# The x loads of the last four batches move from SP's DMA queue to ACT's

## The chip, the cores and the metric

One core of one Trainium2 chip runs the kernel. The metric is the device time of one execution in microseconds, lower is better.

## The reference

Three layers follow one another; everything is float32.

```python
def _attn_ref(x, state):              # x (8, 8, 512, 64), state (8, 8, 32, 64)
    scores = scale * x @ state^T      # softmax over the 32 state rows
    xread = a @ state
    scores2 = scale * state @ x^T     # softmax over the 512 rows of x
    sread = a2 @ x                    # the slot reads
    return concatenate([xread, sread], axis=2)

def _moe_ref(x, phi, w1, w2):         # x (4608, 512), 32 slots, 8 experts
    logits = x @ phi
    d = softmax of logits over the tokens;  slot_input = d.T @ x
    slot_out[e] = relu(slot_input[e] @ w1[e]) @ w2[e]
    c = softmax of logits over the slots;   return c @ slot_out

def _moe2_ref(x, w_gate, w_output_gate, w1, w2):   # top 1 of 8 experts, two gates
    out[mask] = gate_w * eom * (relu(x[mask] @ w1[e]) @ w2[e])
```

## The kernel before, in words

**Stages.** Attention comes first, one batch of x (1 MB) per step. Then the sums over tokens of the first expert layer, its eight matrices w1 and its eight w2 (2 MB each), then the gates and the sorting of tokens by expert of the second layer, and last a loop over 34 to 41 tiles of 128 tokens, with the second layer's matrices held in SBUF. The kernel is written with one hand-ordered program per engine (SP, GpSimd, TensorE, ScalarE = ACT, VectorE) and semaphores between them. There is no planner: each engine's order is the order of its code.

**Buffers.** `arena` and `parts` hold ten slots of 2 MB. x uses the slots 6 and 7 as four buffers `x_sb[0..3]` (a batch b is in buffer b % 4), so x of batch 4 may be loaded when batch 0 has been read for the last time. The last reader is TensorE's `slot_reads` (line 604), which counts up `rd_psum`; the other reader is the copy of x into the layout `xr` (line 288, `lay_x`, on VectorE for batches 0 and 1, on GpSimd from 2 on), which counts up `x_laid`. The matrices of the first expert layer are numbered u = 0 to 15 (w0 to w15 here), those of the second from 16 on. w0 to w3 have slots that nothing used before, w4 waits for `rd_psum` of 6, w5 for the last scores, w6 for `rd_psum` of 8, w7 for the last logits, w8 and w9 for `u_psum`, which TensorE gives behind attention; from w10 on each waits until its slot's matrix has been used. The first eight are loaded in four pieces of 512 KB, in which each of 128 partitions gets 4 KB at a stretch. A load of x has stretches of 1 KB, the state loads (`load_state`, line 293, eight of 64 KB) of 256 B.

**One step k of attention.** TensorE turns the scores of batch k - 2 (`turn_scores`, lines 565 and 571, two halves), turns x of batch k (`turn_x`, line 541, four groups of four transposes), turns the weights of batch k - 3 (line 582), computes the scores of batch k - 1 (line 554), the logits of batch k - 3 (line 589) and the slot reads of batch k - 2 (line 604). ACT in step k: for each of two halves the copy of the turned scores of batch k - 2 out of PSUM (line 905) and two copies of turned x (line 911); then exponentials (921), the logits' copy (927), and the exponential and the copy of the scores of batch k - 1 (938, 942). TensorE needs `xr` of batch k for line 541, GpSimd makes it with line 288 as soon as x has landed and the four groups of the batch before have been turned. GpSimd's line 432 (the normalised weights of batch k - 2) stands behind line 288 of batch k + 1.

**SP** issues nearly all loads, in one order:

```python
            load_w(0)
            load_x(4)
            load_w(1)
            load_x(5)
            load_w(2)
            for i in range(2):
                load_state(e, i)
            load_x(6)
            load_w(3)
            load_x(7)
            e.wait_ge(rd_psum, NB - 2)
```

`load_x(b)` waits, for b of 4 to 7, for `rd_psum` and `x_laid` of b - 3, and so everything behind it on SP waits too. ACT issues one DMA in the whole kernel before the change, the table of tokens (line 1006).

Of the kernel before, what the change touches and what calls it, by code (L numbers as in the profile page):

```python
# [27 lines left out]
NB, NH, S, NS, D = 8, 8, 512, 32, 64  # L28
# [3 lines left out]
J = S // P  # L32
# [22 lines left out]
def last_user(u):  # L55

    before = [v for v in range(u) if SLOT[v] == SLOT[u]]
    return before[-1] if before else None


def build(nc, x, state, phi, w1, w2, wgate, wogate, v1, v2, out, table):
    with ExitStack() as ctx:
# [3 lines left out]
        def sem(name):  # L66
            return ctx.enter_context(nc.semaphore(name))
# [8 lines left out]
        def slot(k):  # L76
            if k < NE:
                return arena[:, k * UNIT:(k + 1) * UNIT]
            return parts[:, (NE + 1 - k) * UNIT:(NE + 2 - k) * UNIT]


        x_sb = [arena[:, 6 * UNIT + 2048 * q:6 * UNIT + 2048 * (q + 1)] for q in range(4)]
# [103 lines left out]
        x_laid, gates_in = sem("x_laid"), sem("gates_in")  # L186
        small_in, phi_in, rows_in = sem("small_in"), sem("phi_in"), sem("rows_in")
        x0_in, x0_laid, x_in = sem("x0_in"), sem("x0_laid"), [sem(f"x_in{q}") for q in range(4)]
# [10 lines left out]
        rd_psum, lgt_psum, lgt_copied = sem("rd_psum"), sem("lgt_psum"), sem("lgt_copied")  # L199
# [41 lines left out]
        def pieces(u):  # L241

            return 4 if u < EARLY else 1
# [46 lines left out]
        def load_state(e, i):  # L290

            for g in range(G):
                e.dma_start(state_n[32 * g:32 * g + 32, :, 64 * i:64 * i + 64],
                            state[:, 2 * g + i, :, :].rearrange("b n d -> n b d")).then_inc(small_in, 16)
# [9 lines left out]
        def wait_used(e, u):  # L304

            if u < 2 * NE:
                e.wait_ge(w_used, u + 1)
            else:
                e.wait_ge(g_psum, u + 1 - 2 * NE)
# [4 lines left out]
        @block.sync  # L314
        def _(e):
            e.dma_start(state_rows, state.rearrange("b h (f t) d -> (b h f) (t d)", f=2)).then_inc(rows_in, 16)
            half = NH // 2
            x0 = x[0].rearrange("h (p j) d -> p h (j d)", j=J)
            x0_sb = x_sb[0].rearrange("p (h c) -> p h c", h=NH)
            e.dma_start(x0_sb[:, 0:half, :], x0[:, 0:half, :]).then_inc(x0_in, 16)  # L320
            e.dma_start(x0_sb[:, half:NH, :], x0[:, half:NH, :]).then_inc(x_in[0], 16)
            e.dma_start(phi_sb[:, :, :], phi.rearrange("(g p) e -> p g e", p=P)).then_inc(phi_in, 16)

            def load_x(b):
                if b >= 4:
                    e.wait_ge(rd_psum, b - 3)
                    e.wait_ge(x_laid, b - 3)
                e.dma_start(x_sb[b % 4].rearrange("p (h c) -> p h c", h=NH),
                            x[b].rearrange("h (p j) d -> p h (j d)", j=J)).then_inc(x_in[b % 4], 16)

            def load_w(u):
                v = last_user(u)
                if v is not None:
                    wait_used(e, v)
                src, ex, _ = w_dram[u]
                rows = src[ex].rearrange("(p c) n -> p (c n)", p=P)
                step = UNIT // pieces(u)
                for a in range(0, UNIT, step):
                    e.dma_start(slot(SLOT[u])[:, a:a + step], rows[:, a:a + step]).then_inc(w_in[SLOT[u]], 16)

            for b in range(1, 4):
                load_x(b)
            e.wait_ge(no_row_ready, 2)
            e.dma_start(table[0:FIRST_ROW, :], no_row[:, :]).then_inc(table_out, 16)
            e.dma_start(wg_sb[:, :, 0:NE], wgate.rearrange("(p c) e -> p c e", p=P)).then_inc(gates_in, 16)
            e.dma_start(wg_sb[:, :, NE:2 * NE], wogate.rearrange("(p c) e -> p c e", p=P)).then_inc(gates_in, 16)
            load_w(0)
            load_x(4)
            load_w(1)
            load_x(5)  # L350
            load_w(2)
            for i in range(2):
                load_state(e, i)
            load_x(6)
            load_w(3)
            load_x(7)
            e.wait_ge(rd_psum, NB - 2)
            e.wait_ge(x_laid, NB - 2)
            load_w(4)
            e.wait_ge(st_psum, 2 * NB)  # L360
            load_w(5)
            e.wait_ge(rd_psum, NB)
            e.wait_ge(x_laid, NB)
            load_w(6)
            e.wait_ge(lgt_psum, NB)
            load_w(7)
            e.wait_ge(u_psum, 2)
            for u in range(8, NU):
                load_w(u)
            for ex in range(NE):  # L370
                wait_used(e, max(v for v in range(NU) if SLOT[v] == ex))

                if ex >= 2:
                    e.wait_ge(v2_in[ex - 1], 16)
                    e.sem_inc(v2_ready, 1)
                e.dma_start(slot(ex).rearrange("p (c n) -> p c n", c=CF),
                            v2[ex].rearrange("(c p) n -> p c n", p=P)).then_inc(v2_in[ex], 16)
                if ex == 1:
                    e.wait_ge(v2_in[0], 16)
                    e.sem_inc(v2_ready, 1)  # L380
            e.wait_ge(v2_in[NE - 1], 16)
            e.sem_inc(v2_ready, 1)
# [508 lines left out]
        def _(e):  # L891
# [5 lines left out]
            for k in range(STEPS):  # L897
                for i in range(2):
                    if 0 <= k - 2 < NB:

                        m = 2 * (k - 2) + i
                        e.wait_ge(e2_psum, m + 1)
                        if k - 2 >= 1:
                            e.wait_ge(rd_psum, k - 2)
                        e.activation(e2[i], pE[:, :].rearrange("p (j c) -> p j c", j=J), ACT.Copy)\
                         .then_inc(e2_copied, 1)
                    for g in (2 * i, 2 * i + 1) if k < NB else ():
                        e.wait_ge(xt_psum, G * k + g + 1)
                        if k >= 2:
                            e.wait_ge(st_psum, 2 * (k - 1))  # L910
                        e.activation(xT[k % 2][:, g, :], pX[g % 2][:, :], ACT.Copy).then_inc(xt_copied, 1)  # L911
                if k == 2:
                    e.wait_ge(pre_psum, 3)
                    for i in range(2):
                        e.activation(pcat[:, :, i, :], pPhi[i][:, 0:NB * NS].rearrange("p (b e) -> p b e", b=NB),
                                     ACT.Copy, scale=1.0 / SCALE).then_inc(pre_copied, 1)
                for i in range(2):
                    if 0 <= k - 2 < NB:
                        m = 2 * (k - 2) + i
                        e.wait_ge(sub_done, m + 1)  # L920
                        e.activation(ew[i], ew[i], ACT.Exp).then_inc(ew_ready, 1)

                def keep_across(b):
                    e.wait_ge(lgt_psum, b + 1)
                    if b >= 1:
                        e.wait_ge(lg_psum, b)
                    e.activation(lgT, pT[:, 0:P], ACT.Copy).then_inc(lgt_copied, 1)

                if 3 <= k < STEPS - 1:
                    keep_across(k - 3)  # L930
                for i in range(2):
                    if 0 <= k - 1 < NB:
                        b = k - 1
                        m = 2 * b + i
                        e.wait_ge(nb_ready, m + 1)
                        if b >= 1:
                            e.wait_ge(e2_psum, m - 1)
                        e.activation(e2T[i], pS[i][:, :], ACT.Exp, bias=nbias[:, i:i + 1],
                                     accum_out=sum2[:, b, i:i + 1]).then_inc(e2t_ready, 1)
                        if b >= 1:  # L940
                            e.wait_ge(r_psum, m - 1)
                        e.activation(sT[i], pS[i][:, :], ACT.Copy).then_inc(st_copied, 1)
                if k in (NB, STEPS - 1):

                    q = int(k > NB)
                    e.wait_ge(srt_psum, q + 1)
                    e.activation(srT[:, q, :, :].rearrange("p g (b n) -> p b g n", b=4),
                                 pX[q][:, :].rearrange("p (b g n) -> p b g n", b=4, g=G),
                                 ACT.Copy).then_inc(srt_copied, 1)
                if k == STEPS - 1:  # L950
                    keep_across(k - 3)
# [410 lines left out]
```

## Time and profile before

| | |
|---|---|
| time, median of 3 runs | 486.56 us (485.65 to 487.3) |
| profiled execution: its time | 489.24 us |
| profiled execution: span | 487.5 us |
| mean granted TensorE clock | 0.961 |
| TensorE matmul busy | 432.2 us (89%) |
| VectorE, ACT, GpSimd busy | 143.4, 124.1, 123.6 us |
| moved by DMA | 87.27 MB, 179 GB/s over the span |

The profile is one execution. Busy time is that of the matmuls as modelled, and does not show what is waited for; the chain that ended last and the idle time in front of an instruction do. In rows of the timeline the first number is the start in microseconds from the span's start, the second the time from the first of the merged instructions to the end of the last, `x4` their number, and the bracket behind them the idle time of that engine before them with what ended it. SPq is SP's sequencer, which issues DMAs; the time beside it is that of issuing and not of the transfer.

### The profile page before, as it was taken

To read this page: it belongs to the slowest core of one execution; us is meant where nothing else is said; L and a number is where in the kernel's file an instruction comes from. 1 tells how busy PE (TensorE), PEld (TensorE's weight loads), DVE (VectorE), ACT (ScalarE), POOL (GpSimd) and SP (SyncE) were. 2 spreads that over 40 slices of the span, in tenths; PEclk is the share of its full clock that TensorE was granted. 3 is DMA by queue.
4 is the path that set the end of the run, shared out by engine and by line. 5 is a ranking of instruction groups with operands and counts; after the bars stand their busy time and mean duration, and the time that the engine had idled before them with its cause. 6 is when DMAs were issued, how large, how long until landed. Compare 5 with 4: busy or idle time off the path is not lost.

```text
span 487.5 us, 9528 instructions
## 1 busy us (share of the span) xinstructions
PE 432.2 (89%) x3474; PEld 229.3 (47%) x3475; DVE 143.4 (29%) x410; ACT 124.1 (25%) x329; POOL 123.6 (25%) x190
## 2 busy tenths in 40 slices
PE   7869786599877957799999999999999999999991
PEld 5657564474315524444444444444444444444440
DVE  2579789850000782102111110101011110101000
ACT  3868675221000200112112121212112121212100
POOL 2343332104000003023242323323242323323110
PEclk9999999989998858799999999999999999999997
DMA  8979909669999999766782101011010101011110
GB/s 286 285 260 300 346 18 327 219 223 428 429 428 428 428 425 386 272 225 212 244 285 89 45 23 46 23 46 42 26 44 24 46 23 45 23 46 44 23 48 2
DMA packets 31710, 87.27 MB, mean 179 GB/s; under 512 B 6140, under 2 KB 14908, under 8 KB 29628
## 3 DMA queue, kind: packets, MB, share of 16 engines
q1 hardware_dynamic: 27580, 76.66, 42.7%
q0 software_dynamic: 3952, 9.54, 5.9%
q8 instruction: 24, 0.39, 0.3%
q10 hardware_dynamic: 144, 0.59, 0.3%
q14 instruction: 10, 0.08, 0.0%
HBM read 77.27 MB, written 9.78 MB: 179 GB/s over the span
## 4 chain that ended last, share of the span: by engine, by line
PE 70%; DMA 18%; DVE 5%; issue 3%; ACT 1%; POOL 1%; SPq 0%; POOLq 0%; DVEq 0%; ACTq 0%
PE bank L868 51%; DMA arena<-in_moe_w 12%; DMA arena<-in_x 6%; PE bank L855 5%; PE bank L753 3%; PE bank L771 1%; PE bank L541 1%; PE bank L530 1%; PE bank L554 1%; PE bank L848 1%; POOL z L288 1%; PE bank L582 1%; PE bank L804 1%; PE bank L690 1%; PE bank L571 1%
## 5 line engine op out<-in xcount | busy, mean ns | idle before, releaser
L868 PE MATMUL bank<-arena,z 128*128 x560 | 251.9, 603 | 0.0
L868 PEld LDWEIGHTS bank<-arena,z 128*128 128x128 f32 x560 | 104.5, 191 | 123.5 <-issue 119.5
L1321 DVE TENSOR_SCALAR z<-bank 128x256 f32<-128x256 f32 x70 | 26.5, 420 | 222.9 <-PE bank L855 222.9
L1032 ACT ACTIVATE z<-bank,gate_to 128x512 f32<-128x512 f32 x35 | 24.0, 687 | 224.3 <-PE bank L868 224.3
L480 POOL DMA_INDIRECT out<-z,rows_to x35 | 36.1, 1033 | 29.9 <-POOL rows_to L477 29.9
L477 POOL CAST rows_to<-gate_to 128x1 int32<-128x1 f32 x35 | 6.4, 184 | 146.5 <-ACT z L1032 146.5
L460 POOL DMA_INDIRECT z<-token_rows,rows_from x32 | 33.6, 1049 | 25.6 <-POOL rows_from L467 25.6
L804 PE MATMUL bank<-arena,soT 128*32 128x256 f32 x224 | 19.6, 510 | 9.3 <-DMA arena<-in_moe_w 8.5
L855 PEld LDWEIGHTS bank<-cT,parts 32*128 32x128 f32 x560 | 19.2, 189 | 16.7 <-issue 16.6
L855 PE MATMUL bank<-cT,parts 32*128 32x128 f32 x560 | 25.9, 300 | 0.0
L541 PE MATMUL bank<-ident,z 128*128 128x128 f32 x128 | 17.0, 275 | 7.6 <-POOL z L288 5.5
L1024 ACT ACTIVATE z<-bank 128x256 f32<-128x256 f32 x70 | 23.0, 388 | 1.1 <-PE bank L855 1.1
L460 POOL DMA_INDIRECT z<-token_rows,sidx x4 | 4.2, 1054 | 71.5 <-DVE sidx L1290 70.6
L288 POOL COPY z<-arena 128x2048 f32<-128x2048 f32 x6 | 11.4, 1894 | 39.1 <-DMA arena<-in_x 24.9
L432 POOL TENSOR_TENSOR parts<-z,rrec 128x512 f32<-128x512 f32 x16 | 16.4, 1047 | 17.5 <-DVE rrec L1103 17.4
L911 ACT ACTIVATE arena<-bank 128x512 f32<-128x512 f32 x32 | 17.5, 602 | 11.5 <-PE bank L541 11.4
L541 PEld LDWEIGHTS bank<-ident,z 128*128 128x128 f32 x128 | 14.1, 140 | 9.8 <-POOL z L288 6.2
L771 PE MATMUL bank<-arena,z 128*32 128x512 f32 x96 | 12.2, 650 | 5.7 <-DMA arena<-in_moe_w 5.7
L804 PEld LDWEIGHTS bank<-arena,soT 128*32 128x32 f32 x224 | 8.3, 138 | 18.1 <-DMA arena<-in_moe_w 10.5
L530 PE MATMUL bank<-ident 128*128 128x128 f32 x86 | 15.1, 337 | 1.6 <-POOL ident L389 1.6
L530 PEld LDWEIGHTS bank<-ident 128*128 128x128 f32 x86 | 12.9, 179 | 4.0 <-issue 2.5
L753 PE MATMUL bank<-arena,z 128*32 128x512 f32 x128 | 14.1, 594 | 0.0
(202 smaller groups left out, 398.5 us busy)
## 6 DMA issues: line engine op xcount, KB each, us to landing
arena<-in_moe_w SPq DMA_DIRECT2D x21, 2048.0 KB, 21.6
arena<-in_moe_w SPq DMA_DIRECT2D x32, 512.0 KB, 6.9
arena<-in_x SPq DMA_DIRECT2D x7, 1024.0 KB, 6.9
parts<-in_moe_w SPq DMA_DIRECT2D x3, 2048.0 KB, 12.9
arena<-in_x SPq DMA_DIRECT2D x2, 512.0 KB, 5.8
token_rows<-z ACTq DMA_DIRECT2D x1, 578.0 KB
out<-z,rows_to POOLq DMA_INDIRECT x35, 2.9
z<-in_state SPq DMA_DIRECT2D x1, 512.0 KB, 3.5
```

The lines of the kernel that those rows point to most:

```text
L460: e.indirect_dma_start(row[q], None, table, bass.IndirectOffsetOnAxis(ap=rows, axis=0), bounds_check=last_row, oob_is_err=False).then_inc( ...
L480: e.indirect_dma_start(out, bass.IndirectOffsetOnAxis(ap=rows_to[:, q % 2:q % 2 + 1], axis=0), ysb[q % 2], None, bounds_check=last_out, oo ...
L530: e.transpose(to[:, 0:P], ident[:, :], ident[:, :])
L541: mm = e.transpose(pX[g % 2][:, P * j:P * j + P], xr[:, j, P * g:P * g + P], ident[:, :])
L753: mm = e.matmul(pX[fh][32 * c:32 * c + 32, :], siTm[:, P * u + NS * c:P * u + NS * c + NS], w[:, c, 512 * fh:512 * fh + 512], start=(u == ...
L804: mm = e.matmul(pG[ex % 4][32 * q:32 * q + 32, 0:GW], soT[:, c, 0:NS], w[:, c, GW * q:GW * q + GW], start=(c == 0), stop=(c == CD - 1))
L855: mm = e.matmul(bank[g][:, P * h:P * h + P], gNow[p][32 * g:32 * g + 32, P * h:P * h + P], cT[p][32 * g:32 * g + 32, :], start=True, stop= ...
L868: mm = e.matmul(pY[p][:, :], hT[p][:, c, :], arena[:, bass.ds(ex * UNIT + 512 * c, 512)], start=(c == 0), stop=(c == CF - 1))
L911: e.activation(xT[k % 2][:, g, :], pX[g % 2][:, :], ACT.Copy).then_inc(xt_copied, 1)
L1024: a = e.activation(hT[p][:, 2 * g:2 * g + 2, :], bank[g][:, 0:GW].rearrange("p (c t) -> p c t", c=2), ACT.Relu)
L1032: e.activation(ysb[p], pY[p][:, :], ACT.Copy, scale=gate_to[:, q, 0:1])\
L1321: v = e.tensor_scalar(hT[p][:, 2 * g:2 * g + 2, :], bank[g][:, 0:GW].rearrange("p (c t) -> p c t", c=2), 0.0, None, ALU.max)
```

## The change

SP's `load_x` loses its two waits and is called for batches 1 to 3 only. The loads of x of batches 4 to 7 are issued by ACT, in step k = 3 to 6 for batch k + 1, behind the wait for the slot reads of batch k - 3 that ACT has there in any case and before the first copy of line 905; a wait for `x_laid` is added in front of each. SP's order becomes w0, w1, w2, the state loads, w3, then w4 with its waits as before.

```diff
             def load_x(b):
-                if b >= 4:
-                    e.wait_ge(rd_psum, b - 3)
-                    e.wait_ge(x_laid, b - 3)
                 e.dma_start(x_sb[b % 4].rearrange("p (h c) -> p h c", h=NH),
                             x[b].rearrange("h (p j) d -> p h (j d)", j=J)).then_inc(x_in[b % 4], 16)
...
             load_w(0)
-            load_x(4)
             load_w(1)
-            load_x(5)
             load_w(2)
             for i in range(2):
                 load_state(e, i)
-            load_x(6)
             load_w(3)
-            load_x(7)
             e.wait_ge(rd_psum, NB - 2)
...
                         e.wait_ge(e2_psum, m + 1)
                         if k - 2 >= 1:
                             e.wait_ge(rd_psum, k - 2)
+                        if i == 0 and 4 <= k + 1 < NB:
+                            e.wait_ge(x_laid, k - 2)
+                            e.dma_start(x_sb[(k + 1) % 4].rearrange("p (h c) -> p h c", h=NH),
+                                        x[k + 1].rearrange("h (p j) d -> p h (j d)", j=J)).then_inc(x_in[(k + 1) % 4], 16)
                         e.activation(e2[i], pE[:, :].rearrange("p (j c) -> p j c", j=J), ACT.Copy)\
                          .then_inc(e2_copied, 1)
```

## Rows read from the trace of the kernel before

**Rows 1.** The page, part 4: the chain that ended last, by engine.

```profile
PE 70%; DMA 18%; DVE 5%; issue 3%; ACT 1%; POOL 1%; SPq 0%; POOLq 0%; DVEq 0%; ACTq 0%
```

**Rows 2.** That chain in order of time: start us, us, what.

```profile
35.53 6.87 DMA arena<-in_x
...
51.04 11.97 DMA arena<-in_x
...
137.55 36.26 DMA arena<-in_moe_w
```

**Rows 3.** Timeline of TensorE, 34 to 72 us: transposes of x (L541).

```profile
34.83 0.65 PE L604 MATMUL bank<-arena 128*32 128x64 f32 x31 [3.43 <-issue]
...
36.44 1.04 PE L541 MATMUL bank<-ident,z 128*128 128x128 f32 x8
...
44.39 1.09 PE L541 MATMUL bank<-ident,z 128*128 128x128 f32 x8 [0.44 <-POOL z L288]
...
55.27 1.09 PE L541 MATMUL bank<-ident,z 128*128 128x128 f32 x8 [2.98 <-POOL z L288]
...
65.03 1.10 PE L541 MATMUL bank<-ident,z 128*128 128x128 f32 x8 [2.11 <-POOL z L288]
```

**Rows 4.** Timeline of SP, 0 to 200 us: the DMA issues.

```profile
13.78 3.01 SPq L339 DMA_DIRECT2D arena<-in_moe_w  x4
24.38 0.38 SPq L328 DMA_DIRECT2D arena<-in_x  x1
...
35.53 0.38 SPq L328 DMA_DIRECT2D arena<-in_x  x1
...
38.80 8.00 SPq L293 DMA_DIRECT2D z<-in_state  x8
46.90 1.35 SPq L328 DMA_DIRECT2D arena<-in_x  x1
48.29 2.56 SPq L339 DMA_DIRECT2D arena<-in_moe_w  x4
51.04 0.38 SPq L328 DMA_DIRECT2D arena<-in_x  x1
```

**Rows 5.** Timeline of GpSimd, 10 to 100 us: a copy of x (L288).

```profile
53.33 1.89 POOL L288 COPY z<-arena 128x2048 f32<-128x2048 f32 x1 [6.97 <-DMA arena<-in_x]
```

**Rows 6.** Timeline of ACT, 10 to 66 us: line 905, first half, steps 3 to 6.

```profile
25.40 0.65 ACT L905 ACTIVATE arena<-bank 128x512 f32<-128x512 f32 x1
...
36.21 0.60 ACT L905 ACTIVATE arena<-bank 128x512 f32<-128x512 f32 x1 [2.64 <-PE bank L565]
...
44.26 0.63 ACT L905 ACTIVATE arena<-bank 128x512 f32<-128x512 f32 x1
...
52.61 0.62 ACT L905 ACTIVATE arena<-bank 128x512 f32<-128x512 f32 x1
```

**Rows 7.** DMA packets, MB, share: 38 to 40, 46 to 48, 170.5 to 176 us.

```profile
q1 hardware_dynamic: 710, 0.74, 105.8%
...
q1 hardware_dynamic: 1267, 0.39, 126.1%
...
q1 hardware_dynamic: 121, 1.72, 74.2%
q10 hardware_dynamic: 116, 0.54, 23.7%
```

**Rows 8.** Line 328, the x loads of SP: issue (ns min/median/max) and landing.

```profile
L328 SPq DMA_DIRECT2D arena<-in_x x7: 378/602/3375, 2.8 to 51.0; - x7
...
DMA to landing us min/median/max: 6.3/6.9/11.1
```

**Rows 9.** Stretches: length, busy PE PEld DVE ACT POOL, PEclk, DMA share, GB/s.

```profile
20.00:22.00 2.00, 2.00 (x25) 0.92 (x23) 1.38 (x2) 1.69 (x5) 0.89 (x1) 1.00 1.03 416
23.50:25.50 2.00, 1.67 (x30) 1.58 (x30) 1.90 (x6) 2.00 (x7) 1.19 (x2) 1.00 0.05 18
32.00:36.00 4.00, 1.18 (x36) 1.08 (x37) 1.74 (x7) 1.57 (x4) 2.64 (x3) 1.00 0.67 263
...
171.00:173.00 2.00, 0.00 (x0) 0.00 (x0) 2.00 (x12) 0.06 (x1) 0.00 (x0) 1.00 0.99 412
173.00:183.00 10.00, 7.19 (x64) 2.77 (x64) 8.51 (x47) 0.38 (x1) 0.00 (x0) 0.50 1.01 429
```

## The prediction

> **What bounds the kernel now.** I read the page first. The chain that ended last is mostly TensorE (the output matmuls at its end) with 18% DMA in it [rows 1]. Those 18% are of two kinds, which the chain in order of time separates: short pieces in the attention phase, where a transfer of x is waited for, and long ones behind 137 us, where the expert weights are [rows 2]. The change touches the first kind. The weights from the ninth on are requested only when matmuls behind the attention phase have run, so they start later or earlier exactly as that phase ends, and a microsecond won or lost in attention arrives whole at the end.
>
> So the question is when attention ends. Its steps are best read at one instruction, the first transposes of x of a batch (line 541), which stand at 36.44, 44.39, 55.27 and 65.03 us for batches 4 to 7. Ahead of the last three TensorE idled 0.44, 2.98 and 2.11 us for GpSimd's copy of x (line 288) [rows 3]. Without these waits the steps are 7.51, 7.90 and 7.65 us: I take 7.7. The copies themselves waited for the DMA (the queue's own rows are the next to read): TensorE goes on 1.94 us after a copy starts, as 53.33 to 55.27 shows [rows 3, 5].
>
> Why were they late? x6 was issued at 46.90, because SP spent 8.00 us before it on eight small loads of state; ACT reaches its line 905 of that step at 44.26 [rows 4, 6]. x7 was issued at 51.04 behind w3 in the same queue and was not there until 63 [rows 2, 4]. x4 and x5 stand ahead of w1 and w2 in the queue and were nearly in time. A transfer of x that meets nothing takes 6.3 us from issue to landing [rows 8].
>
> **What the change removes.** SP's four waits and four issues go, at 0.38 us or more each [rows 8]; nothing waits for SP itself. The best case follows from the waits alone: 0.44 + 2.98 + 2.11 = 5.5 us, less what the issue on ACT costs.
>
> **What it adds on ACT.** Four issues ahead of the copy of line 905, one in each of the steps that began it at 25.40, 36.21, 44.26 and 52.61 [rows 6]. No row shows a load issued on ACT; the same load took SP 378 ns at least, 602 in the median and 3375 at most, where earlier transfers still filled its queue [rows 8]. A gain of time is excluded, so the cost is 0.38 to 3.4 us each; ACT's queue is empty each time, so I take 0.38. Behind the issue stand the copy and, through it, TensorE's next transposes. For x4 and x5 TensorE will be waiting anyway (below), so these hide; for x6 and x7 I charge 0.1 each. The new waits are old ones or long met (the copy of batch k-3 out of the buffer), and cost nothing.
>
> **What it moves.** x4 goes from 24.38 to 25.4, x5 from 35.53 to 36.2, x6 from 46.90 to some 44, x7 from 51.04 to 52.6 on the old clock. But SP's other loads are moved too, past four waits each: w1, w2, the eight state loads and w3 no longer queue behind an x. SP finished w0's issue at 16.8 [rows 4], so all of them are requested from then on. Before, the DMA engines idled after w0 (18 GB/s from 23.50 to 25.50 [rows 9]) and x4 came first out of the pause. Now w1 stands there, and x4 must share.
>
> How two queues share, the trace shows in one place: 121 packets of SP's queue went beside 116 of ACT's in 5.5 us, 1.72 and 0.54 MB [rows 7]. They alternate packet by packet, whatever the size. That is bad for x: its packets are 1 KB, those of w 4 KB. Per engine (16 of them) a w packet takes 4096 B / (416 GB/s / 16) = 0.158 us [rows 9], an x packet 2 us x 16 / 710 = 0.045 [rows 7], a state packet of 256 B 2 x 16 / 1267 = 0.025 [rows 7]. x has 64 packets per engine, w 32 per matrix of 2 MB, the state loads 128 in all. A turn beside w costs 0.203 us, beside state 0.070.
>
> **x4.** Of the 6.3 us alone, 64 x 0.045 = 2.9 are data; I put 1.9 ahead of them (the pause ended at about that distance from the issue) and 1.5 behind. First packet 25.4 + 1.9 = 27.3. w0 ends about 6.2 us behind its last issue, at 23.0 (the DMA is idle soon after [rows 9]); w1 and w2 of 2.10 MB / 416 GB/s = 5.05 us each would end at 33.1. So 5.8 us or 36 w packets are left: 36 x 0.203 = 7.3, to 34.6. The other 28 go beside state, 2.0, to 36.6. Landing 38.1, TensorE 40.0 in place of 36.44.
>
> **x5.** Issued at 36.2, whatever x4 does (its wait is for the scores and reads of batch 1); first packet 38.1. State packets left then: 128 - 28 - 1.5/0.025 = 40, so 40 x 0.070 = 2.8, to 40.9; 24 go beside w3, 4.9, to 45.8. Landing 47.3, TensorE 49.2; the step alone would allow 40.0 + 7.7 = 47.7.
>
> **x6, x7.** ACT stands at line 905 some 8.0 us behind the first transposes (44.26 - 36.44 = 7.8, 52.61 - 44.39 = 8.2 [rows 3, 6]): x6 at 48.0, when w3 is through. Alone it needs 6.3 + 1.94: 56.2; the step allows 49.2 + 7.7 = 56.9. x7 at 57.2, TensorE 65.4. With 0.1 twice: 65.6 against 65.03.
>
> **Sum:** batch 4 +3.6, batch 5 +4.8, batch 6 +1.6, batch 7 +0.5 us; the two ends of the chain nearly cancel. The profiled execution took 489.24 (span 487.5), so it would read about 489.7; it lies 2.7 above the median of 486.56, and on that median the sum is 487.0. Bounds: x5 needs only 0.8 us less to cost nothing over its step, and an x4 held up by 2 us less brings 2 us; so this case alone covers 485.0 to 489.0.
>
> **Rivals.** (1) *x is hardly held up.* If the weights' packets come slower than I take it once SP's queue is full, or the shared row [rows 7] is no measure for loads, x4 and x5 land as alone: TensorE 36.4 for batch 4, 44.4, 52.7, 60.6 for batch 7, with the issue costs 60.8: 4.2 us faster, 482.3. For it: the waits of rows 3 do go. The Trainium skill (DMA: Bandwidth & Descriptors, Issuing engines are not separate DMA queues) says that starting transfers from several engines saves only the time to issue them, as all interleave on the same engines. By that rule the gain is bounded by x6's 46.90 - 44.26 = 2.6 us, and it speaks against this change; the packet counts above agree with it.
>
> (2) *x5 is the last out of the backlog.* Place: step of batch 5. All data ahead (x5 itself, 100 state packets, w3) ends at 36.6 + 2.9 + 2.5 + 5.05 = 47.1; if x5's packets start by 38.9 or later, state is gone, every turn is beside w3, and it ends there: landing 48.6, TensorE 50.5, batch 7 at 66.9: 1.9 slower, 488.5; with x4 also 1.5 later (a longer start behind a full queue) 490. It decides from where batch 5 starts behind 50.2. The gap of 3.43 us in line 604, which nothing in the profile explains [rows 3] and which fell in w1's transfer, could come a second time and leads to the same side.
>
> (3) *The clock.* TensorE was busy 1.18 of 4 us around that gap and the granted clock stayed 1.00 (2.4 GHz), yet 173 to 183, behind at least 2 us without any matmul, ran at 0.50 (1.2 GHz) [rows 9]. If the longer wait for x4 drops it, the step behind it, 7.5 of 8 us TensorE, stretches by about half of the time at the low level: up to 1.7 us, 488.7. The Trainium skill (TensorE: Matmul & The Clock Gate, Why this matters for your kernels) warns that a gap between bursts throttles the clock again; the first row disagrees, the second agrees.
>
> **Chances.** Forecast 0.50, (1) 0.20, (2) 0.24, (3) 0.06. A measurement of this kernel tells 0.3% (1.5 us) from no change. The forecast's own spread puts 0.2 of it on faster, 0.6 on same, 0.2 on slower: 0.10, 0.30, 0.10. (1) goes to faster but for 0.01. (2) goes to slower but for 0.04, (3) half and half. Faster 0.30, same 0.37, slower 0.33. The range for 8 in 10 runs from (1), 482.3, to (2) with its late x4, 490. The likeliest case's own is 485.0 to 489.0.
>
> **What would show it.** Four loads of x on ACT's queue; SP done with w3's issue before 36. No pause of the DMA behind w0. The copies of line 288 for batches 4 to 7 at about 38, 47, 55 and 63. Batch 4's transposes near 40, the waits for batches 6 and 7 under 1 us. If x4 lands before 35 the sharing is wrong; if batch 4 starts in time and the gain is missing, look at ACT's issues. Behind 65 us every stage must keep its length, or the step that carries attention's time to the end is wrong.

## The result: 1.4% slower

| | before | changed |
|---|---|---|
| time, median | 486.93 us (4 runs) | 493.03 us (4 runs) |
| ratio | | 1.0136, 95% interval 1.0104 to 1.0169 |
| profiled execution: time, span | 489.24, 487.5 us | 492.43, 490.6 us |
| mean granted TensorE clock | 0.961 | 0.958 |

487.0 was predicted, with a range from 482.3 to 490. The kernel lost 6.1 us, and the two profiles differ by 3.2 only. The first experiment clears that up: the profiled execution of before was an unlucky one, with a pause that others don't have.

The profile after, in the order of the prediction's steps. The timeline of SP, 13 to 100 us:

```profile
14.60 8.64 SPq L336 DMA_DIRECT2D arena<-in_moe_w  x12
23.28 14.47 SPq L293 DMA_DIRECT2D z<-in_state  x8
37.80 61.48 SPq L336 DMA_DIRECT2D arena<-in_moe_w  x20
```

w0, w1 and w2 are requested by 23.2 us, the state loads by 37.8 (they took 14.5 us to issue and not 8.0 [rows 4]; in experiment 8, where hardly anything stood in front of them, 4.7). The issues of x on ACT:

```profile
24.98 0.45 ACTq L900 DMA_DIRECT2D arena<-in_x  x1
34.05 0.38 ACTq L900 DMA_DIRECT2D arena<-in_x  x1
51.32 0.37 ACTq L900 DMA_DIRECT2D arena<-in_x  x1
59.85 0.38 ACTq L900 DMA_DIRECT2D arena<-in_x  x1
```

An issue on ACT costs what it does on SP with an empty queue. GpSimd's copies of x for batches 4 to 7:

```profile
40.35 1.89 POOL L288 COPY z<-arena 128x2048 f32<-128x2048 f32 x1 [13.68 <-DMA arena<-in_x]
...
47.67 1.89 POOL L288 COPY z<-arena 128x2048 f32<-128x2048 f32 x1 [3.41 <-PE bank L534]
...
56.70 1.89 POOL L288 COPY z<-arena 128x2048 f32<-128x2048 f32 x1 [3.35 <-DMA arena<-in_x]
...
65.13 1.89 POOL L288 COPY z<-arena 128x2048 f32<-128x2048 f32 x1 [3.25 <-DMA arena<-in_x]
```

x4 took 15.4 us from issue to copy (15.3 to its landing), where 6.3 had been the least from issue to landing [rows 8]; x6 and x7, which meet nothing, took 5.4 and 5.3 to their copies. TensorE's first transposes of x, which answer to [rows 3]:

```profile
42.30 1.97 PE L534 MATMUL bank<-ident,z 128*128 128x128 f32 x8 [7.85 <-POOL z L288]
...
51.61 1.04 PE L534 MATMUL bank<-ident,z 128*128 128x128 f32 x8
...
60.14 1.04 PE L534 MATMUL bank<-ident,z 128*128 128x128 f32 x8
...
68.67 1.04 PE L534 MATMUL bank<-ident,z 128*128 128x128 f32 x8
```

Two things are to be seen. Batch 4 waits 7.85 us and its transposes then take 1.97 us in place of 1.04, at half clock. And from batch 5 on nothing waits for x any more, yet the steps are 8.53 us, twice to the hundredth, not the 7.7 that I had used. What sets them stands in the chain that ended last, between 49 and 55 us (start, us, what):

```profile
49.64 0.68 DVE nbias L1088
50.32 0.62 DVE rsum L1098
...
51.13 0.66 DVE rsum L1098
...
51.98 0.40 DVE rs L1128
...
52.81 0.28 DVE z L1138
53.09 0.61 DVE rmx L1067
...
53.72 0.70 DVE z L1071
...
54.56 0.63 PE bank L564 x4
55.19 0.87 PE bank L534 x8
```

It is VectorE's chain, into which TensorE's four pieces (L564, L534, L575, L547) are strung.

### The profile page after: what moved, and what is told of

It is laid out like the page before. It is cut to its first block, busy times and chain, and to the rows that moved or that the text cites. A ratio compares the mean times of both kernels' runs of the same rounds, so it can differ in the third digit from the quotient of the medians.

```text
span 490.6 us, 9524 instructions
## 1 busy us (share of the span) xinstructions
PE 432.3 (88%) x3474; PEld 229.1 (47%) x3475; DVE 144.1 (29%) x410; ACT 123.8 (25%) x329; POOL 123.6 (25%) x190
## 4 chain that ended last, share of the span: by engine, by line
PE 69%; DMA 17%; DVE 6%; issue 2%; ACT 2%; POOL 1%; SPq 0%; DVEq 0%; POOLq 0%; ACTq 0%
PE bank L861 51%; DMA arena<-in_moe_w 12%; DMA arena<-in_x 5%; PE bank L848 5%; PE bank L746 3%; PE bank L764 2%; PE bank L534 1%; DVE rsum L1098 1%; DVE rmx L1067 1%; PE bank L564 1%; PE bank L547 1%; PE bank L841 1%; PE bank L575 1%; PE bank L683 1%; DVE z L1071 1%
## 5 line engine op out<-in xcount | busy, mean ns | idle before, releaser
L534 PE MATMUL bank<-ident,z 128*128 128x128 f32 x128 | 17.7, 284 | 10.3 <-POOL z L288 7.8
L288 POOL COPY z<-arena 128x2048 f32<-128x2048 f32 x6 | 11.3, 1891 | 38.2 <-DMA arena<-in_x 31.0
L534 PEld LDWEIGHTS bank<-ident,z 128*128 128x128 f32 x128 | 14.9, 146 | 12.0 <-POOL z L288 8.1
L575 PE MATMUL bank<-ident,parts 128*128 128x128 f32 x64 | 10.3, 286 | 5.7 <-DVE z L1138 5.3
L523 PE MATMUL bank<-ident 128*128 128x128 f32 x86 | 13.4, 308 | 1.6 <-POOL ident L382 1.6
```

The costliest lines, as they stand in the source:

```text
L534: mm = e.transpose(pX[g % 2][:, P * j:P * j + P], xr[:, j, P * g:P * g + P], ident[:, :])
```

## The experiments

Two theories stood at the start. **Theory 1:** x4 shares the DMA engines with w1, w2 and the state loads, packet by packet. **Theory 2:** the issue on ACT is what costs. Two side questions: the clock, and the baseline.

**1. The kernel before once more** (no edit, one run).

> The kernel before, unchanged, for a second profile. In the first profile TensorE had an unexplained gap of 3.43 us in line 604 of the fourth step, and that execution took 489.24 us against a median of 486.93. Theory A: the gap is an accident of one execution; here it is under 1.5 us and batch 4's transposes start 2 to 3 us earlier than 36.44, time about 487. Theory B: the gap belongs to the kernel and is here again at 3.4 us.

486.38 us. Theory A holds: line 604 has no such gap, and in none of the twelve other profiles of this study is the gap in front of batch 4 above 1.8 us. TensorE's transposes, batches 4 to 7:

```profile
33.27 1.04 PE L541 MATMUL bank<-ident,z 128*128 128x128 f32 x8
...
41.92 1.09 PE L541 MATMUL bank<-ident,z 128*128 128x128 f32 x8
...
53.50 1.97 PE L541 MATMUL bank<-ident,z 128*128 128x128 f32 x8 [2.67 <-POOL z L288]
...
63.35 1.09 PE L541 MATMUL bank<-ident,z 128*128 128x128 f32 x8 [0.94 <-POOL z L288]
```

An ordinary execution starts batch 4 at 33.3 and batch 7 at 63.4. The changed kernel is late against that by 9.0 us at batch 4 and 5.3 at batch 7, and its time by 492.43 - 486.38 = 6.05. The row of batch 6 shows half clock (1.97 us) behind a wait of 2.67 us; in the first profile the clock had stayed up through the pause of 3.43 and a wait of 2.98 us [rows 3, 9]. So the length of a wait alone doesn't tell whether the clock falls.

**2. x alone.** ACT still issues x4 to x7; SP holds back the rest.

```diff
             load_w(0)
+            e.wait_ge(x_in[3], 32)
             load_w(1)
```

> The changed kernel, but SP waits until x7 has landed before it requests w1, w2, the state loads and w3. ACT still issues x4 to x7. Theory 1 (the loss comes from sharing the DMA engines with w1, w2 and state): x4 lands 6.3 us behind its issue, at about 31.3, batch 4 starts near 33.5, the steps are the 8.53 us that the changed kernel shows when it waits for nothing, batch 7 near 59.5: 9 us earlier than in the changed kernel, about 484 us. Theory 2 (issuing on ACT is what costs): x lands early but the time stays within 2 us of the changed kernel's 493.

482.62 us, ratio to before 0.9904 (0.9869 to 0.9939). x4's copy and the first transposes of batches 4 and 7:

```profile
31.41 1.89 POOL L288 COPY z<-arena 128x2048 f32<-128x2048 f32 x1 [5.21 <-DMA arena<-in_x]
...
34.82 1.04 PE L535 MATMUL bank<-ident,z 128*128 128x128 f32 x8
...
59.23 1.04 PE L535 MATMUL bank<-ident,z 128*128 128x128 f32 x8
```

Theory 2 is out: with the same four issues on ACT the kernel is 10 us faster than the changed one, and faster than before.

**3. SP's old pace.** The two waits in front of each x load come back on SP, without the loads.

```diff
             load_w(0)
+            old_wait(4)    # rd_psum and x_laid of 1, and so on
             load_w(1)
+            old_wait(5)
             load_w(2)
...
+            old_wait(6)
             load_w(3)
+            old_wait(7)
```

> The changed kernel with SP's old waits kept in their old places, without the x loads: w1, w2, w3 are requested when they were before. ACT issues x4 to x7. Theory 1 (sharing): x4 meets w1 alone, all its turns beside 4 KB packets for about 6 us, and lands near 35.5; batch 4 starts near 37.5, x6 meets state and w3. In all 1 to 3 us slower than before, 488 to 490, well ahead of 493. Theory 2 (ACT's issue costs): 492 or more.

496.42 us, 1.0162 (1.0116 to 1.0209), beside 1.0136 (1.0104 to 1.0169) for the changed kernel: not told apart from it by these intervals. Theory 1's number, 488 to 490, missed; taken alone, the time fits theory 2's ("492 or more"). The profile shows that it is not the issue that costs. TensorE's two long waits:

```profile
41.64 1.97 PE L542 MATMUL bank<-ident,z 128*128 128x128 f32 x8 [9.09 <-POOL z L288]
...
65.75 1.97 PE L542 MATMUL bank<-ident,z 128*128 128x128 f32 x8 [6.09 <-POOL z L288]
```

x4, issued at 24.09, was copied at 39.70 and not at 35.5. Its packets had gone sooner; ACT's queue from 24.5 to 34 and from 34 to 36 us:

```profile
q10 hardware_dynamic: 958, 0.97, 34.6%
...
q10 hardware_dynamic: 68, 0.07, 9.3%
```

Those are 1,026 packets. x4 has 1,040, 1,024 of data and one short one on each of the 16 DMA engines, which counts the semaphore up; x5, issued at 32.10, stands behind it in the same queue, so the count alone doesn't say whose they are. The trace's events of x4's semaphore do: 15 of the DMA engines had reported by 35.50 us and the last one at 39.64. One was late by 4 us, and a load has landed when its slowest engine is through. w2 had been requested in SP's queue from 31.3 us on. And x6, issued at 50.67, met w3, which SP had issued at 49.87 on the same event, and was copied at 63.81: 13.1 us where the changed kernel, in which w3 was long through, took 5.4. One matrix in flight in the other queue is enough. ACT's issues took 0.37 to 0.45 us here too, as in experiment 2, so theory 2 gains nothing from the 496.

**4. All on SP, x first.** The same as 2, with who issues x undone.

```diff
             load_w(0)
             load_x(4)
-            load_w(1)
             load_x(5)
-            load_w(2)
-            for i in range(2):
-                load_state(e, i)
             load_x(6)
-            load_w(3)
             load_x(7)
+            load_w(1)
+            load_w(2)
+            for i in range(2):
+                load_state(e, i)
+            load_w(3)
```

> The kernel before, all on SP, with w1, w2, the state loads and w3 moved behind x7; ACT issues nothing. It differs from the run in which x was alone on ACT's queue only in who issues x. If who issues matters little (theory 1), the time is within 2 us of that run's 482.6; x4 is issued when the reads of batch 0 are done, x6 some 2 us earlier than ACT could. If issuing on ACT is itself worth something, this one is slower than that run by 2 us or more.

482.48 us, 0.9905 (0.9883 to 0.9928), equal to experiment 2. Its transposes:

```profile
32.65 1.04 PE L541 MATMUL bank<-ident,z 128*128 128x128 f32 x8
...
41.18 1.04 PE L541 MATMUL bank<-ident,z 128*128 128x128 f32 x8
...
49.71 1.04 PE L541 MATMUL bank<-ident,z 128*128 128x128 f32 x8
...
58.24 1.04 PE L541 MATMUL bank<-ident,z 128*128 128x128 f32 x8
```

No wait for x, and three steps of 8.53 us. The late weights do not show in the time.

**5. w3 ahead of the state loads** (in the changed kernel: `load_w(3)` moved up behind `load_w(2)`; one run).

> The changed kernel with w3 ahead of the state loads. Theory 1a (packets of the two queues alternate one for one, so the size of what x meets decides): all 64 turns of x4 are beside 4 KB packets, 64 x 0.203 = 13.0 us from 28.7, landing near 43 and batch 4 near 45, 2.5 us behind the changed kernel's 42.30. Theory 1b (x4 must let through whatever was requested ahead of it, in bytes): w1 and w2 are ahead in both, so x4 lands at 40.3 as there.

```profile
45.46 1.97 PE L534 MATMUL bank<-ident,z 128*128 128x128 f32 x8 [11.03 <-POOL z L288]
```

x4's copy starts at 43.51 and batch 4 at 45.46; the time is 498.70. Theory 1a had 43 and 45, theory 1b 40.3. What came behind w2 in the other queue decided, though w1 and w2 were ahead in both.

**6. Smaller packets** (in the changed kernel, w1 and w2 in eight pieces; one run, 493.89 us).

```diff
-            return 4 if u < EARLY else 1
+            return 8 if u in (1, 2) else 4 if u < EARLY else 1
```

> The changed kernel with w1 and w2 loaded in eight pieces of 256 KB, so in stretches of 2 KB in place of 4. Theory 1a: a turn costs 0.079 + 0.045 = 0.124 us, 64 turns 7.9 us from 28.7; x4 lands about 38.3 and not 40.3. Theory 1b: the bytes ahead are the same, 40.3 stays.

Half right. Packets, MB and share by queue from 30 to 34 us (q1 is SP's, q10 ACT's), first of the changed kernel:

```profile
q1 hardware_dynamic: 331, 1.22, 77.2%
q10 hardware_dynamic: 331, 0.34, 24.7%
```

and with pieces of half the size:

```profile
q1 hardware_dynamic: 524, 0.96, 66.6%
q10 hardware_dynamic: 518, 0.53, 38.8%
```

The queues move the same number of packets, whatever their size, and x moves 1.56 times as fast (0.203 / 0.124 = 1.64 was expected). But x4's copy started at 40.28, as in the changed kernel (40.35). Of x4's 1,024 packets 925 had gone by 36 us, against 758 in the changed kernel, and still the last of the 16 DMA engines reported at 40.23 us, against 40.30 there. So the rule of turns holds for the bulk of a load, and not for its landing, which the slowest engine makes. Theory 1b's number came out and its reason did not: experiment 5 had spoken against it. Why that engine is late stayed open.

**7. x4 alone protected.** As 2, with SP waiting for x4 only (`e.wait_ge(x_in[0], 32)`; one run).

> The changed kernel with SP waiting for x4 to have landed before it requests w1, w2, state and w3. Batch 4 starts as in the run with x alone, near 34.8. x5, issued on ACT some 3 us behind the landing, now meets w1 and w2: start about 3.7 behind its issue at 34.5, 64 turns of 0.203 = 13.0, and 3 us for the slowest engine: lands near 54, batch 5 near 56, worse than in the changed kernel (51.6). So protecting one x alone moves the loss to the next: 495 or more.

494.68 us. Batch 4 at 34.22, then x5, issued at 33.98, copied at 49.90, batch 5 at 51.84: the loss of the changed kernel, one batch later. The landing was 4 us sooner than worked out. The sum had put every turn beside a 4 KB packet; in the trace 531 of x5's 1,024 packets had gone by 45 us, and most of the rest went beside the state loads' packets of 256 B, which SP's queue moved from there on.

**8. State and w3 late.** The kernel before with only these two moved behind x7.

> The kernel before with only the state loads and w3 moved behind x7; w1 and w2 stay where they are, behind x4 and x5 in the same queue. If a load that is queued behind an x in the same queue does it no harm, this is as good as the run with all of them behind x7: batch 4 at 33, then steps of 8.5, 482.5. If w1 and w2 in flight hurt x5 and x6 it keeps part of the old waits: 484 to 486.

485.70 us, 0.9970 (0.9939 to 1.0001): inside the expected 484 to 486, with an interval that just reaches no change. Batch 5 still waits:

```profile
43.37 1.09 PE L541 MATMUL bank<-ident,z 128*128 128x128 f32 x8 [2.21 <-POOL z L288]
```

x5 was issued at 31.37, with w1 (issued from 23.4 to 27.0) in front of it in its own queue and w2 (from 31.79) behind, and copied at 41.42, 10.05 us later. Fourteen of the 16 DMA engines had reported by 38.28 and the last at 41.37, so here too the slowest engine makes the landing. Matrices in the same queue cost too; whether it is the one in front or the one behind was not separated. x4, which had w1 behind it and only the end of w0 in front, took 7.06 us in this run.

**9 to 11. The clock.** In the changed kernel TensorE is given transposes of the identity while it waits for x4.

```diff
+                if k == 4:
+                    e.wait_ge(xt_copied, G * k - 1)
+                    keep_clock(24, pX[0])    # 36, 68
                 if now:
                     turn_x(k, (0, 1))
```

> The changed kernel with 24 transposes of the identity (4.7 us) put into TensorE's wait for x4; they write a bank that is free then and is overwritten afterwards. Theory 3 (part of the loss is the clock that fell to half at 39.5 us, after 5.6 us of idling): the clock stays at 1.00, batch 4's first transposes take 1.0 in place of 1.97 us, and batch 5 starts about 1.3 us earlier: 491.7. If the step of batch 4 is set by VectorE's chain as the later ones are, the clock costs only the difference 9.31 - 8.53 = 0.8 us.

> As the run with 24 transposes in the wait for x4, with 36 (7.1 us). With 24 TensorE was idle for the last 4 us of the wait and the clock still fell, at 40.9. If the clock is worth anything here: no half clock between 35 and 50 us, batch 5 about 1.0 us earlier against batch 4's start than in the changed kernel (9.31 us there), and a time about 1 us under the changed kernel's. If VectorE's chain sets that step, it stays at or above 8.5.

> The changed kernel with 68 transposes in the wait for x4; 36 of them took 4.1 us, so these take 7.7 and end just before x4 is there. No stretch of half clock between 35 and 50 us; batch 5 starts 8.5 to 8.6 us behind batch 4, not 9.3. If the clock is a real part of the loss, the time is 0.8 to 1 us under the changed kernel's 493.0; the granted clock of that step is the surer sign.

24 and 36 of them were too few: they took 2.8 and 4.1 us, ended 5.5 and 3.1 us before TensorE could go on, and the clock fell all the same (491.92 us, 1.0103, and 493.15 us, 1.0122). With 68 it did not. Stretches of the changed kernel (length, busy PE, PEld, DVE, ACT, POOL, granted clock, DMA, GB/s):

```profile
35.00:39.50 4.50, 0.00 (x0) 0.00 (x0) 0.18 (x1) 0.08 (x1) 0.00 (x0) 1.00 1.14 276
39.50:46.30 6.80, 4.00 (x19) 4.00 (x20) 1.38 (x2) 1.48 (x3) 3.90 (x3) 0.50 1.11 295
```

and with 68:

```profile
35.00:39.50 4.50, 4.50 (x43) 4.50 (x42) 0.00 (x0) 0.00 (x0) 0.00 (x0) 1.00 1.08 324
39.50:46.30 6.80, 4.96 (x44) 4.48 (x42) 2.43 (x4) 2.38 (x5) 4.07 (x4) 1.00 1.12 288
```

The starts of batches 4 and 5 with 68:

```profile
42.59 1.09 PE L534 MATMUL bank<-ident,z 128*128 128x128 f32 x8 [1.84 <-POOL z L288]
...
50.08 1.16 PE L534 MATMUL bank<-ident,z 128*128 128x128 f32 x8
```

That is 7.49 us in place of 9.31, so the low clock, 1.2 GHz of 2.4, cost 1.8 us of that step. The times don't show it: 491.56, 1.0103 (1.0063 to 1.0144) beside 1.0136 is the right direction with intervals that overlap, and the run with 24 transposes, in which the clock fell, has the same ratio of 1.0103. The price rests on the granted clock and the step in the profiles.

The 7.49 also explains my 7.7: behind a long wait VectorE has caught up, and the one step that follows is short. In that step TensorE waits for VectorE nowhere; in the steps of 8.53 us it does twice, 0.59 and 0.26 us.

**12. One VectorE instruction less**, on top of 4.

```diff
-                        e.tensor_scalar(rs2[:, b, :], sum2[:, b, :], EPS, None, ALU.add).then_inc(sr_step, 1)
-                        e.wait_ge(sr_step, 2 * b + 1)
-                        e.reciprocal(rs2[:, b, :], rs2[:, b, :]).then_inc(sr_step, 1)
-                        e.wait_ge(sr_step, 2 * b + 2)
+                        e.reciprocal(rs2[:, b, :], sum2[:, b, :]).then_inc(sr_step, 1)
+                        e.wait_ge(sr_step, b + 1)
```

> All loads on SP, x first (the run of 482.5 us), and VectorE's addition of 1e-9 to the sums of the slot softmax left out (line 1131; the sums are at least 1, so float32 does not see it), one instruction of 0.40 us per step. Theory V (once x is there, VectorE's chain sets the step at 8.53 us): the steps become 8.1 us, batch 7's transposes come 1.3 us earlier against batch 4's, and over the whole phase the kernel gains 2 to 3 us: 480. Theory T (TensorE's 7.7 us is the step and 8.53 comes from elsewhere): nothing changes.

478.61 us, 0.9834 (0.9792 to 0.9876), the best of the study and ahead of both kernels. Its transposes of batches 5 and 6:

```profile
41.09 1.04 PE L541 MATMUL bank<-ident,z 128*128 128x128 f32 x8
...
49.14 1.04 PE L541 MATMUL bank<-ident,z 128*128 128x128 f32 x8
```

Batch 7's stand at 57.19. These are two steps of 8.05 us: 8.53 - 8.05 = 0.48 for an instruction of 0.40. VectorE's chain is the step. The time gained is 3.9 us against experiment 4, above the 2 to 3 expected. By the end of attention it is 2.7 (the first matmuls of line 680 stand at 89.41 us and, in experiment 4, at 92.09); the rest was not traced.

## Why the prediction was wrong, point by point

The step that failed is the one from the waits to the last batch: batch 7 was to start 0.5 us later than before, and started 5.3 us later. Three terms of it were mis-sized, x4's landing, the baseline and the 7.7 us of a step; a fourth, the pace behind x4, came out right by luck.

- **"Are x4 and x5 held up, and how":** right in kind. The two queues move equal numbers of packets (331 beside 331), and the issue on ACT costs 0.4 us and hides. A turn beside w was worked out at 0.203 us; 4 us x 16 / 331 gives 0.193.
- **x4's landing, 38.1:** mis-sized by 2.2 us; it landed at 40.30. Its first packet moved at 28.6, not 27.3 (from 25 to 28 us 345 of SP's queue went and none of ACT's), 3.6 us behind the issue where x6 and x7, alone, needed 1.1, so the 1.9 fitted neither. And 1.5 us were charged for the end, while the 16 DMA engines reported from 37.28 to 40.30 us, 3.0 us apart. Neither can be read from loads that meet nothing.
- **The baseline of batch 4, 36.44:** wrong, and at batch 4 the largest error. 3.2 us of it were the gap in line 604, which belonged to one execution (33.27 in the second profile). The wait for x4 hides such a gap, so I set against the change a pause that an ordinary run does not have: +3.6 was worked out where it is +9.0. The prediction named the gap as unexplained and used it all the same. At batch 7 the same error is 65.03 against 63.35, 1.7 us.
- **"Without these waits the steps are 7.7":** wrong. Taking TensorE's idle time out of a step leaves TensorE's work, not the step. Steps that wait for nothing are 8.53 us (experiments 2 and 4), VectorE's. The gain to be had at batches 6 and 7 was therefore small: before, the two waiting steps take 10.88 and 9.76 us, 3.6 together above 8.53, and not 5.1.
- **x5 (TensorE at 49.2) and rival (2):** not what happened. Batch 5 started at 51.61 because batch 4 had been late and slow; x5 had landed at 45.33, 2 us sooner than forecast, and its copy waited for TensorE. The forecast had 9.2 us between batches 4 and 5, for x5's DMA; the 9.31 measured are the low clock. That they agree is luck. Something like rival (2) does happen once x4 is protected (experiment 7).
- **Rival (3), the clock,** had 6%, and its mechanism and price came true: 1.8 us against the 1.7 worked out. The wait was longer than forecast, 7.85 us. The Trainium skill (TensorE: Matmul & The Clock Gate, Why this matters for your kernels) warns that a gap between bursts of matmuls throttles the clock again, and this trace agrees: 0.50 from 39.5 us on, behind some 5 us without a matmul.
- **Rival (1)** is out. The Trainium skill (DMA: Bandwidth & Descriptors, Issuing engines are not separate DMA queues) says that loads issued from several engines run on the same DMA engines, and that only the time to issue them is saved. That held: 482.48 and 482.62 us with x from SP and from ACT. With nothing beside x the loss is gone (experiments 2 and 4); part of the loss went through the clock, which fell in the wait that the sharing made.
- **The signs:** the DMA did not pause behind w0, and the waits for batches 6 and 7 were gone, as written. SP reached w3's issue only at 37.8 us, not before 36.
- **Behind attention** the premise held: what attention lost arrived at the end. The first transposes behind the last of x (L614 in the second profile of before, L607 here) are 6.1 us apart, and the spans 6.0:

```profile
70.03 0.60 PE L614 MATMUL bank<-ident,z 128*128 128x128 f32 x4
...
76.14 0.60 PE L607 MATMUL bank<-ident,z 128*128 128x128 f32 x4
```

  In front of them 0.8 us come to the 5.3 of batch 7, by the effect of the 7.49: in before batch 7 had waited, and its step to this row took 6.68 us; here it took 7.47. Behind them the distance moves (4.8 us at the first matmuls of line 690, here 683: before ran at a granted clock of 0.50 from 97.4 to 100.7 us) and comes back; where, was not traced.

The sum: the forecast for the median was 487.0 and 493.03 was measured. 1.7 of the 6.0 us are the baseline at batch 7. 3.1 are batch 7 later than forecast (68.67 in place of 65.6), of which x4's landing is 2.2 and the two steps of 8.53 most of the rest. 0.8 is the step behind batch 7, and 0.4 the median of before, which four runs put at 486.93 and not at 486.56. Apart from that, the parts of the chances add up to 0.29, 0.38 and 0.33, not quite to the 0.30, 0.37 and 0.33 given.

## What to carry to other kernels

A wait in front of a load may do a second job: it holds back everything queued behind it. When the load is moved to another queue, that job must be done elsewhere, or the transfer someone is waiting for shares the DMA engines, packet by packet, with megabytes for which nobody waits. Smaller packets beside it sped up its bulk here, but not its landing. And before a gain is read from idle time in front of an engine, look for the chain that comes next, and take two profiles: one accident in one of them moved this sum by 3 us at batch 4 and by 1.7 at batch 7.

## What the runs showed of the hardware that was not expected

- A 1 MB load in stretches of 1 KB, issued on ACT's queue while SP's held w1, w2 and the state loads, took 14.7 to 15.8 us to its copy in five kernels; with nothing beside it, some 5.3 us.
- Its first packet moved 3.6 to 3.8 us behind the issue in these kernels, and 1.1 us behind it with nothing beside it (x6 and x7 of the changed kernel).
- A matrix requested 0.8 us before x6 made it take 13.1 us (experiment 3), not far from the 15.4 of x4 in the changed kernel, which had megabytes queued long before it.
- With packets of both kinds in flight, 15 of the 16 DMA engines can be through with a load 4 us before the last one is (experiment 3).
- TensorE's pause without a releaser in line 604 (597 in the changed kernel) differs between executions: 3.43 us in the first profile, none in the second of the same kernel, and 0 to 1.8 us at this place in the twelve of the other kernels.
